# Eight experts of a top-1 mixture: one width for all, in a straight line, in place of a width for each, in a loop with branches

## The reference, cut to what matters

```python
# 1: attention, B=2, H=8, S=576, D=64, window of 128, with ALiBi bias -> x, 1152 tokens x 512
# 2: top-1 mixture, E=8 experts, capacity = 1152 // 8 * 2 = 288
logits = x @ w_gate
expert_idx = np.argmax(logits, axis=1)
...
for i in range(N):                      # token i goes to the next free row of its expert
    e = expert_idx[i]
    if counts[e] < capacity:
        disp[e, counts[e]] = x[i]; pos[i] = counts[e]; counts[e] += 1; keep[i] = True
h = np.maximum(np.einsum('ecd,edf->ecf', disp, w1), 0.0)     # 512 -> 1024
y = np.einsum('ecf,efd->ecd', h, w2)                         # 1024 -> 512
out[i] = gate_w[i] * y[expert_idx[i], pos[i]]
# 3: feed-forward block, 512 -> 2048 -> 512, with h * sigmoid(h)
```

## Time and profile before

| what | value |
|---|---|
| median of three timed runs | 616.2 us (613.0 to 620.09) |
| the profiled execution, first to last instruction | 616.6 us |
| TensorE busy | 488.1 us (79%) |
| VectorE busy | 324.2 us (53%) |
| ScalarE busy | 240.6 us (39%) |
| GpSimd busy | 186.6 us (30%) |
| mean granted TensorE clock | 0.876 of full speed |

### The profile page before, as it was taken

The page is one execution under the profiler, slowest core; times in us unless marked ns, Lnnn a source line. Parts: engine busy times, 40 slices in busy tenths (PEclk is TensorE's granted clock), DMA queues, the critical chain, the costliest instruction groups (busy, mean ns, idle before and its releaser), DMA issues.

```text
span 616.6 us, 9223 instructions
## 1 busy us (share of the span) xinstructions
PE 488.1 (79%) x2974; PEld 451.6 (73%) x2975; DVE 324.2 (53%) x758; ACT 240.6 (39%) x577; POOL 186.6 (30%) x117
## 2 busy tenths in 40 slices
PE   5999989861779086925794584879999999999994
PEld 4898878651769086915693584869999999899993
DVE  4565667551499649882999296952222222222121
ACT  4766857421346134522453142544322222222121
POOL 2012454428453415260446043456301000010001
PEclk9999989855689668975988696969999999999998
DMA  9989310019594508460839063430000000010001
GB/s 209 274 263 255 97 25 19 18 40 287 74 308 146 178 3 287 158 190 4 252 111 262 10 188 130 162 115 1 0 1 18 34 0 0 0 51 0 0 0 51
DMA packets 54470, 65.06 MB, mean 106 GB/s; under 512 B 31936, under 2 KB 31936, under 8 KB 54368
## 3 DMA queue, kind: packets, MB, share of 16 engines
q1 hardware_dynamic: 52592, 59.08, 32.5%
q0 software_dynamic: 1776, 4.73, 2.1%
HBM read 54.35 MB, written 9.44 MB: 103 GB/s over the span
## 4 chain that ended last, share of the span: by engine, by line
PE 49%; issue 14%; DVE 9%; DVEq 1%; ACT 1%; POOL 0%; ACTq 0%; POOLq 0%
PE bank L1063 11%; PE bank L1042 11%; PE bank L1043 11%; PE bank L1044 11%; PE bank L1065 5%; DVE x_lo L854 4%; DVE w_lo L811 2%; DVE x_sum L839 1%; DVE hidden_sum L839 1%; DVE xT L852 1%; PE bank L1048 1%; POOL out_dram L466 0%; DVEq L227 0%; DVE hidden L849 0%; ACTq L227 0%
## 5 line engine op out<-in xcount | busy, mean ns | idle before, releaser
L415 POOL TENSOR_TENSOR w_lo<-w_raw,w_hi 128x1024 fp32r<-128x1024 f32 x56 | 133.6, 2403 | 165.2 <-ACT w_hi L525 165.1
L1063 PE MATMUL bank<-xT,w_hi 128*128 128x320 f32 (+2 forms) x256 | 84.3, 408 | 87.9 <-issue 78.8
L1063 PEld LDWEIGHTS bank<-xT,w_hi 128*128 128x128 f32 x256 | 56.3, 240 | 89.8 <-issue 80.2
L883 DVE TENSOR_TENSOR g_full<-bank,sigmoid 128x384 f32<-128x384 f32 x48 | 26.8, 558 | 138.6 <-ACT sigmoid L601 138.6
L525 ACT ACTIVATE w_hi<-w_raw 128x1024 fp32r<-128x1024 f32 x80 | 82.7, 1043 | 0.0
L601 ACT ACTIVATE sigmoid<-bank 128x384 f32<-128x384 f32 x48 | 23.6, 492 | 137.5 <-PE bank L1044 137.5
L1042 PE MATMUL bank<-x_hi,w_hi 128*128 x192 | 66.6, 347 | 6.6 <-DVE x_lo L854 4.1
L1063 PE MATMUL bank<-hidden,w_hi 128*128 128x320 f32 (+2 forms) x256 | 67.4, 345 | 0.0
L839 DVE TENSOR_REDUCE hidden_sum<-bank 128x160 f32<-128x320 f32 (+2 forms) x64 | 30.9, 486 | 67.9 <-PE bank L1063 67.9
L1044 PE MATMUL bank<-x_hi,w_lo 128*128 x192 | 65.7, 342 | 0.0
L1043 PE MATMUL bank<-x_lo,w_hi 128*128 x192 | 65.7, 342 | 0.0
(11 more groups left out here) (124 smaller groups left out, 915.5 us busy)
## 6 DMA issues: line engine op xcount, KB each, us to landing
w_raw<-in_moe_w_dram SPq DMA_DIRECT2D x64, 512.0 KB, 6.2
dispatched<-dispatch_dram SPq DMA_DIRECT2D x9, 576.0 KB, 8.7
dispatch_dram<-zeros SPq DMA_DIRECT2D x4, 1152.0 KB, 8.0
w_raw<-in_moe_w_in_dram SPq DMA_DIRECT2D x8, 512.0 KB, 4.5
w_raw<-in_moe_w_out_dram SPq DMA_DIRECT2D x8, 512.0 KB, 7.3
q_raw<-in_q_dram SPq DMA_DIRECT2D x8, 256.0 KB, 4.6
k_raw<-in_k_dram SPq DMA_DIRECT2D x8, 256.0 KB, 5.0
v_raw<-in_v_dram SPq DMA_DIRECT2D x8, 256.0 KB, 4.9
```

What stands on the lines that cost most here:

```text
L415: nc.gpsimd.tensor_tensor(wlo[s][:, sl], raw[s][:, sl], whi[s][:, sl], ALU.subtract).then_inc(pool_lo, 1)
L883: nc.vector.tensor_tensor(gf[:, f % 2, :], bank[f % 4][:, 0:TB], sig[:, f % 2, :], ALU.mult).then_inc(gf_ready, 1)
L1063: ins = nc.tensor.matmul(both, ah, x[:, :, 0:w], start=first, stop=last)
```

## The change

The code has two widths in place of four: 192 and 288. VectorE finds the largest of the eight counts (`top8`, one more small reduction) and stores it as one integer in place of the eight counts. Each of TensorE, ScalarE and VectorE loads this one number once, ahead of the first expert, and takes one branch: to the eight experts at width 288 if it is over 192, else to the eight experts at width 192. Within each of the two, the eight experts stand in a straight line, with no loop, load or branch between them (but for the load of an expert's offset, which stays). SyncE's and GpSimd's loops over the experts are written out too. The feed-forward loop stays a loop. All semaphore counts are now constants.

```diff
-    WIDTHS = (128, 160, 192, C)
+    NARROW = 192
...
-        def by_count(eng, e, steps):
-
-            n = count_of(eng, e)
-
-            def either(lower, upper):
-                with eng.If(n > lower):
-                    steps(upper)
-                with eng.Else():
-                    steps(lower)
-
-            with eng.If(n > WIDTHS[1]):
-                either(WIDTHS[2], WIDTHS[3])
+        def by_top_count(eng, experts):
+
+            n = eng.value_load(top[0:1, 0:1], min_val=0, max_val=C)
+            with eng.If(n > NARROW):
+                experts(C)
             with eng.Else():
-                either(WIDTHS[0], WIDTHS[1])
+                experts(NARROW)
...
-            with sp.Fori(0, E // 2 - 1) as j:
-                refill(2 * j, 0)
-                refill(2 * j + 1, 2)
+            for e in range(E - 2):
+                refill(e, 2 * (e % 2))
...
-            with pool.Fori(0, E // 2) as j:
-                share_of_lows(2 * j, 2)
-                share_of_lows(2 * j + 1, 0)
+            for e in range(E):
+                share_of_lows(e, 2 - 2 * (e % 2))
...
-            nc.vector.tensor_copy(counts[:], kept8[:]).then_inc(offs_ready, 1)
+            link(nc.vector.reduce_max(top8[:], kept8[:], axis=AX.X))
+            nc.vector.tensor_copy(top[:], top8[:]).then_inc(offs_ready, 1)
             nc.vector.tensor_copy(offs[:], off8[:]).then_inc(offs_ready, 1)
...
-            with pe.Fori(0, E // 2) as j:
-                expert(2 * j, 2 * STEPS * j + KC, 0)
-                expert(2 * j + 1, 2 * STEPS * j + KC + STEPS, 2)
+            def experts(w):
+                for e in range(E):
+                    steps(w, e, STEPS * e + KC, 2 * (e % 2))
+
+            by_top_count(pe, experts)
```

More of the change, by code:

```diff
@@ L103, in build @@
     offs, o = at("offs", [P, E], I32, o)
-    counts, o = at("counts", [P, E], I32, o)
+    top, o = at("top_count", [P, 1], I32, o)
     permsb, o = at("permsb", [P, N // P], I32, o)
@@ L155, in build @@
     zero8, o = at("zero8", [P, E], F32, o)
+    top8, o = at("top8", [P, 1], F32, o)
     oo, o = at("oo", [P, NTOK, E], F32, o)
@@ L220, in halves @@
             return ([] if t % NT == 0 else [(0, P)]) + [(1, ROWS[t])]
-        def count_of(eng, e):
-            return eng.value_load(counts[0:1, bass.ds(e, 1)], min_val=0, max_val=C)
         def offset_of(eng, e):
             return eng.value_load(offs[0:1, bass.ds(e, 1)], min_val=0, max_val=N)
-        def by_count(eng, e, steps):
-            n = count_of(eng, e)
-            def either(lower, upper):
-                with eng.If(n > lower):
-                    steps(upper)
-                with eng.Else():
-                    steps(lower)
-            with eng.If(n > WIDTHS[1]):
-                either(WIDTHS[2], WIDTHS[3])
+        def by_top_count(eng, experts):
+            n = eng.value_load(top[0:1, 0:1], min_val=0, max_val=C)
+            with eng.If(n > NARROW):
+                experts(C)
             with eng.Else():
-                either(WIDTHS[0], WIDTHS[1])
+                experts(NARROW)
         DVE_LOWS = (0, 2, 4)
@@ L568, in _ @@
             act.wait_ge(offs_ready, 2)
-            def expert(e, first, w_slot, rounds):
-                by_count(act, e, lambda w: steps(w, e, first, w_slot, rounds))
             def steps(w, e, first, w_slot, rounds):
@@ L590, in steps @@
                         weight_high(w_slot + p // PIECES, p % PIECES, rounds)
-            with act.Fori(0, E // 2) as j:
-                expert(2 * j, 2 * STEPS * j + KC, 2, 16 * j + 16)
-                expert(2 * j + 1, 2 * STEPS * j + KC + STEPS, 0, 16 * j + 32)
+            def experts(w):
+                for e in range(E):
+                    steps(w, e, STEPS * e + KC, 2 - 2 * (e % 2), 16 * (e // 2) + 16 * (e % 2) + 16)
+            by_top_count(act, experts)
             def sigmoid(tb, f):
@@ L822, in _ @@
             dve.wait_ge(offs_ready, 2)
-            def expert(e, first, w_slot, splits):
-                by_count(dve, e, lambda w: steps(w, e, first, w_slot, splits))
             def steps(w, e, first, w_slot, splits):
@@ L871, in steps, with experts @@
                 low(STEPS - 1, *order[-1], off)
-            with dve.Fori(0, E // 2) as j:
-                expert(2 * j, 2 * STEPS * j + KC, 2, 4 * PIECES * j + 2 * PIECES)
-                expert(2 * j + 1, 2 * STEPS * j + KC + STEPS, 0, 4 * PIECES * j + 4 * PIECES)
+            def experts(w):
+                for e in range(E):
+                    steps(w, e, STEPS * e + KC, 2 - 2 * (e % 2), 2 * PIECES * (e + 1))
+            by_top_count(dve, experts)
             def g_full(tb, f):
@@ L1074, in _ @@
                 turn_slots(c, bank[c]).then_inc(step_done, 1)
-            def expert(e, first, slot):
-                by_count(pe, e, lambda w: steps(w, e, first, slot))
             def steps(w, e, first, slot):
```

## The result

The changed kernel takes **568.07 us** (three runs, 566.55 to 572.05) against 616.2: 0.925 of the time before (95% interval 0.914 to 0.936). 562 was forecast, with a range of 551 to 577. The profiled execution took 568.07 us, with a span of 566.3 us, 50.3 less than before; the mean granted clock rose from 0.876 to 0.937.

The account below looks back on a forecast made before the run. TensorE waiting for code after jumps was taken as the bound in the expert stage. Entry 6.0 plus jumps 58.3, less widening 9.0 and 7 x 0.1 for the period, gave 54.6 us off 616.6: 562 us, range 551 to 577.

Parts of the forecast that it names:

- The mechanism: Expert stage: TensorE's idle stretches ahead of experts are waits for code after jumps; beyond the residuals, 58.3 us to save.
- the entry: TensorE's way into expert 0: one jump left of two, taken as 5.1 us, 6.0 us less, first up step at 151.7.
- The first expert, sized 24.05 us and the release: Expert 0 at width 192: 24.05 us from first up step to second residual, then 0.14 us until TensorE starts.
- The period, sized 24.3: Time from one expert's second residual to the next, VectorE nearly full: 24.3 us, seven times.
- the end of 25.3: Upper end of the forecast expert period, where VectorE's idle time stays whole (25.28 us).
- The feed-forward stage, sized 216.0: Stage after the experts: claimed unchanged at 216.0 us.
- The widening, sized 9.0: Six experts run at 192, four from 160 and two from 128: 9.0 us more.
- The clock: TensorE's clock may stay up across shorter gaps, sparing it 3.0 us an expert; worth counted inside the period's ends.
- The price list behind the forecast: Idle gaps ahead of experts matched to jump counts: about 5 us per jump to code that is not the next.
- My own subtraction: TensorE's start on each next stage or expert minus VectorE's second residual: 59.4 us over eight places, 58.3 beyond the release.

## Why the prediction was right, and where it was off

*The mechanism held.* TensorE was waiting for code: with the jumps gone, so are all "issue" waits but the one at the entry. The transfers of the kernel before say the same. These are its instruction queues (packets, MB, share) in the 16.64 us of idle time ahead of expert 2, and below them in the 20.85 us of work that follow:

```profile
q8 instruction: 5, 0.08, 2.8%
q14 instruction: 7, 0.06, 2.0%
...
q8 instruction: 2, 0.03, 0.8%
```

The eight idle stretches hold 23 packets of the first queue in 87 us; the whole stage after, from 151.79 to 352.68, holds 10 in 201 us. Which engine a packet is for, the trace does not say. That VectorE's second residual would be the next to release TensorE and that VectorE would be nearly full came as written for experts 1 to 4, and the entry kept one jump of 4.91 us, so that the first up step came within 0.1 us.

*The first expert, sized 24.05 us and the release, took 26.10.* What failed is that the entry was priced on TensorE alone: the jump that stays there is on VectorE as well. Without it the expert took 22.94 us. That is 1.9 us of the miss. By the runs it is VectorE's second stop that counts, not its late first sum: with all residuals on VectorE and the same entry, the first sum followed 3.75 us behind TensorE, no second stop came, and the expert took 21.41 us, against 21.13 with the narrow copy first. Why the second stop came in the one kernel and not in the other stays open.

*The period, sized 24.3, was 24.97 on the mean of seven,* (352.68 - 177.89) / 7, and that is 4.7 us. I had taken 1.1 us of TensorE's late start off expert 5's period of 25.28. TensorE does start sooner, 0.05 us behind the residual (174.46 + 3.38 against 177.89), but VectorE was then the bound, and its own busy time rose by 0.83, from 23.65 to 24.48. Only where its second residual began ahead of GpSimd's did a period come near the forecast (24.38, 24.79, 24.43). The last, up to the feed-forward stage's first matmul, took 26.02, above the end of 25.3: behind a wait of 1.87 us for `hidden` TensorE ran at a granted clock of 0.51 for 6.7 us (341.27 to 348.00), and VectorE stood 1.69 us for it.

*The feed-forward stage, sized 216.0, took 213.6 from its first matmul:* 2.4 us less, of which 1.5 lie ahead of the fourth group of products and 0.9 behind it. Waits for `x_lo` are 0.8 of it (3.24 us against 3.00 and 1.07); over the rest TensorE's clock was higher, 1.00 up to 358.00 where it had been 0.73 and then 0.50. With the entry's 0.1 the parts are 0.1 + 1.9 + 4.7 - 2.4 = 4.3, the profiled span of 566.3 against 562.0. So the forecast came closer than its parts, since one miss made up for half of another.

*The widening, sized 9.0,* measured 7.9 between two kernels without branches. With the jumps left in it was 15.5 (630.85 against 615.37), of which 4.9 are more waiting for code (83.7 against 78.8).

*The clock* neither stayed up nor fell far: 1.00 in expert 1, 0.93 in experts 2 to 6, 0.87 in the last. Its cost stayed within the ends of the period but for that last one.

*The price list behind the forecast was wrong as a rule, though right as a sum.* "A jump to code that is not the next costs about 5 us" is refuted by four kernels: one jump forward per expert cost nothing that shows in the changed kernel and 1.9 us where TensorE had no other wait, the way back of a two-body loop cost nothing either, and the way back in the kernel before cost about 10 us. My own subtraction had shown it: beyond the residual's wait, one jump stood open for 1.2 us, two for 3.3 and 8.8, three for 14.3 and 14.2, four for 16.3. The first is nearly covered, by that wait and, as I read it, by the matmuls still queued; what stands in the open are the further ones of a row. Their number alone is no price: two in a row stood for 5.6 to 12.4 us in the kernel before and in its straight-line form. The 5.1 us for the entry took one jump as 4.6 to 5.6, and the 5.6 was the gap ahead of expert 3, where the same list counts two; that 4.91 came out is in part luck. The Trainium skill, in "Runtime: NRT & Kernel Launch" (Instruction fetch mechanics), says that a branch to a target outside the pages held forces the fetch first. The 32 packets of code against 20 agree, and the 567.78 us beside 568.07 add that such a fetch can be free. The forecast was not hurt, because it took the gaps as wholes and never had to price one jump by itself, but for the entry.

Open: why the order of VectorE and GpSimd slipped into the better pattern between experts 3 and 4 and not before, and why a way back costs about 10 us in one kernel and nothing in the other. How much of the jump's cost is TensorE's own and how much comes through ScalarE's and VectorE's jumps was not separated, since all three had it in every run.

## What to carry to other kernels

Count the jumps that follow one another with no work between them, not the jumps: rows of two to four stood in the open here for 5.6 to 19 us, while one jump per expert, or a short loop's way back, was free as long as another wait lay over it. Take the price from a gap of the same kind, since the count alone does not give it. Before sizing what comes after a stall, look at which engine is nearly full beneath it; here it was VectorE, whose own instructions lasted longer beside GpSimd, and taking the work away from GpSimd gave nearly as much again (0.925 to 0.865) as the change. Where a stage starts behind a jump, price the jump on every engine and not only on the one that starts first.

## What the runs showed that I had not expected

- VectorE's elementwise work on two operands in SBUF lasts far longer while GpSimd makes a residual: `x_lo` 1.87 us on the mean against 0.35, `w_lo` up to 3.4 against 1.2. GpSimd took 2.4 us for each residual that VectorE makes in 1.2, so its help cost more VectorE time than it saved.
- With five more residuals an expert, VectorE is busy for 4.7 us less (19.76 against 24.48), and TensorE's granted clock is 1.00 there, where it was 0.93 in most experts of the changed kernel.
- Code that has run is not always fetched again: the kernel with a loop over two bodies took 15 packets, that with eight bodies in a straight line 20, and the one before, with a loop over eight bodies visited by jumps, 52.
